# A fused linear-attention, ELU MLP and top-1 expert kernel: expert rows loaded in 32-token blocks and turned on VectorE, and two experts' products interleaved across the seam

## The chip, the cores and the metric

The kernel runs on one core of a Trainium2 chip. The core has five engines with instruction streams of their own that meet only through semaphores: TensorE (PE, matrix products into eight PSUM banks), VectorE (DVE), ScalarE (ACT), GpSimd (POOL) and SyncE (SP, which here issues loads), and 16 DMA engines beside them. The metric is the device time of one launch in microseconds (us), lower is better.

## The reference, cut to what matters

```python
x = attention(r, k, v, w, u)             # linear attention with decay, 2 x 768 tokens, 8 heads x 48
x = elu(x @ w_in) @ w_out                # 1536 tokens, 384 -> 2048 -> 384
logits = x @ w_gate                      # 8 experts
e = argmax(logits); gate = softmax(logits)[e]
# expert e takes its tokens in order, into slots disp[e, 0:384]
h = maximum(einsum('ecd,edf->ecf', disp, w1), 0)     # w1: 8 x 384 x 1024
y = einsum('ecf,efd->ecd', h, w2)                    # w2: 8 x 1024 x 384
out[i] = gate[i] * y[e[i], slot[i]]
```

All is fp32. Products are made from fp32r parts: each operand is split in a rounded part (`_hi`) and the rest (`_lo`), and a product is three matmuls, hi x hi, hi x lo and lo x hi.

## The kernel before

The span has three stages: attention by 128-token chunks; the ELU MLP by six blocks of 256 tokens, in which attention chunks, routing and scatter are woven; and from about 265 us the experts. Routing scatters each token's row (384 values of x, the gate, the token's number) into `slots` in HBM, 384 slots for each expert. An expert computes its first 256 slots; a branch at the end that is not taken with these inputs does the overflow.

Expert 0 runs in an order of its own (tiles of 128 slots, `tile_fc1`, `tile_fc2`, `pick_rows`). Experts 1 to 7 run through `expert(i, r, more)`, one function of that name for each engine; expert 2i+r has its weights in buffer r (`EH[r]`, `EL[r]`; the loaded weights `ER[r]` lie in the same bytes as `EL[r]`), its rows in `xrow[r]`. Experts 2 to 5 are a hardware loop.

TensorE, for f from 0 to 7 (an "f step"): FC1 of 128 hidden features, nine matmuls of 256 columns into `ps_e[f % 2]` (L1718 to L1737), then FC2 of step f-2, six matmuls of 384 columns into the two accumulators `ps_ye` (L1697). FC2 of steps 6 and 7 comes at the end of the expert (L1746), so the next expert begins with three FC1 groups in a row. FC1 of step f waits for ge_lo of step f-2 (L1720). Behind FC2 in step 5 TensorE transposes the next expert's rows, six blocks of 128x128, from `xrow` into `ps_xt` (L1684 to L1695).

ScalarE (L935): ge_hi = relu(ps_e) rounded (L940) in each step; the rounded parts of the next expert's w1 in steps 2 to 4 (L945) and w2 in steps 5 to 7 (L953), 1024 columns each; xe_hi from `ps_xt` in step 5. VectorE (L1296): ge_lo in each step (L1301), the rest of w1 in steps 3 to 5 (L1308), xe_lo (L1293) and the token numbers tok_i (L1315) in step 5; at the end the two products with the gate into `yrow` (L1321). GpSimd: the rest of w2 (L724), then two indirect scatters of `yrow` into `out` (L729).

SP issues the loads from one queue in program order (L546 to L554): for expert e = 2i+r

```python
sp.wait_ge(s_he, ET * (2 * i + r + 1))      # all FC1 of expert e done
load_w(2 * i + 2 + r, r)                    # w1 of expert e+2
sp.wait_ge(s_fc2e, ET * (2 * i + r + 1))    # all FC2 of expert e done
load_w2(2 * i + 2 + r, r)
sp.wait_ge(s_ye[r], 2 * (i + 1))            # yrow of expert e done, xrow free
sp.wait_ge(s_tok[r], i + 1)
load_x(2 * i + 2 + r, r)                    # two DMAs of 128 rows of 386 values
```

Of the kernel before, what the change touches and what calls it, by code (L numbers as in the profile page):

```python
# [12 lines left out]
def build(nc, B, H, S, D, DFF, NE, FE, CAP, rkt_in, nat_in, decay, bonus, bonus_pair, win, wout, wouttr, wgate, wexp, out, slots):  # L13
# [5 lines left out]
    DM = H * D  # L19
# [37 lines left out]
    NOVER = NE + 3  # L57
    LATE = NE * CAP
# [39 lines left out]
    x2t = new("x2t", [128, BT, DM])  # L98
    lg = new("lg", [128, BT, NE])
# [32 lines left out]
    def expert_rows(r):  # L132
        return (new(f"xrow{r}", [128, 2, XR]), new(f"xe_hi{r}", [128, KT, SN], F32R),
                new(f"xe_lo{r}", [128, KT, SN], F32R), new(f"yrow{r}", [128, 2, DM]),
                new(f"tok_i{r}", [128, 2, 1], U32))
# [8 lines left out]
    xrow, xe_hi, xe_lo, yrow, tok_i = zip(rows0, expert_rows(1))  # L144
# [32 lines left out]
    with ctx:  # L177
# [223 lines left out]

        def wait_if(eng, s, count):

            if not (isinstance(count, int) and count <= 0):
                eng.wait_ge(s, count)
# [40 lines left out]
        def _(sp):  # L446
# [128 lines left out]
        def _(pool):  # L575
# [143 lines left out]
            def split_w2(e_i, r):  # L719

                for c in range(N1):
# [25 lines left out]
            split_w2(0, 1)  # L747
# [29 lines left out]
        def _(act):  # L777
# [151 lines left out]
            def expert_x(i, r):  # L929

                act.wait_ge(s_xtr[r], i + 1)
                nc.scalar.copy(xe_hi[r][:, 0:2, :], ps_xt[0][:, :].rearrange("p (k n) -> p k n", k=2)).then_inc(s_xehi[r], 1)
                nc.scalar.copy(xe_hi[r][:, 2, :], ps_xt[1][:, 0:SN]).then_inc(s_xehi[r], 1)
# [48 lines left out]
        def _(dve):  # L982
# [273 lines left out]
            def tokens_of(t, s):  # L1256
                dve.wait_ge(s_xr[0], 16 * (t + 1))
                V.tensor_copy(tok_i[0][:, t, :], xrow[0][:, t, TOKEN:XR]).then_inc(s, 1)

            def gated(t, y):  # L1260
                V.tensor_scalar(yrow[0][:, t, :], y, xrow[0][:, t, GATE:GATE + 1], None, ALU.mult).then_inc(s_ye[0], 1)
# [20 lines left out]
            for c in range(N1):  # L1282
# [4 lines left out]
            dve.wait_ge(s_y0, 1)  # L1287
            gated(0, ps_y[0][:, 0:DM])

            def expert_x(i, r):  # L1290
                for c, (src, dst) in enumerate(((ps_xt[0][:, :], (0, 2)), (ps_xt[1][:, 0:SN], (2, 3)))):
                    dve.wait_ge(s_xehi[r], 2 * i + c + 1)
                    V.tensor_tensor(xe_lo[r][:, dst[0]:dst[1], :], src.rearrange("p (k n) -> p k n", n=SN),  # L1293
                                    xe_hi[r][:, dst[0]:dst[1], :].bitcast(F32), ALU.subtract).then_inc(s_xelo[r], 1)

            def expert(i, r, more):  # L1296
                ni, nr = (i, 1) if r == 0 else (i + 1, 0)
                for f in range(ET):
# [4 lines left out]
                                           op1=ALU.subtract).then_inc(s_gelo, 1)  # L1303
                    if more and F_W1 < f <= F_W1 + N1:
# [11 lines left out]
                for t in range(2):  # L1316
                    if t == 0:
                        dve.wait_ge(s_y0, 2 * i + r + 1)
                    else:
                        dve.wait_ge(s_fc2e, ET * (2 * i + r + 1))  # L1320
                    V.tensor_scalar(yrow[r][:, t, :], ps_ye[t][:, 0:DM], xrow[r][:, t, GATE:GATE + 1], None,  # L1321
                                    ALU.mult).then_inc(s_ye[r], 1)

            tile_row(s_he, ET, s_lrow)
# [39 lines left out]
        def _(pe):  # L1364
# [292 lines left out]
            def pick_rows():  # L1657

                pe.wait_ge(s_xr[0], 32)
                for kt in range(KT):  # L1660
                    mm(ps_s[0][:, 128 * kt:128 * kt + 128], xrow[0][:, 1, 128 * kt:128 * kt + 128], ident[:, :],
# [3 lines left out]
                for kt in range(KT):  # L1665
                    for t in range(BT):
                        last = mm(ps_s[0][:, 128 * kt:128 * kt + 128], rows[:, t, NE + 128 * kt:NE + 128 * kt + 128],
# [16 lines left out]
            def expert_x(i, r):  # L1684
                pe.wait_ge(s_xr[r], 32 * (i + 1))
                if r:
                    pe.wait_ge(s_xelo[0], 2 * (i + 1))
                else:
                    wait_if(pe, s_xelo[1], 2 * i)
                for kt in range(KT):  # L1690
                    for t in range(2):
                        at = (kt % 2) * SN + t * 128
                        last = nc.tensor.transpose(ps_xt[kt // 2][:, at:at + 128],  # L1693
                                                   xrow[r][:, t, 128 * kt:128 * kt + 128], ident[:, :])
                last.then_inc(s_xtr[r], 1)  # L1695

            def fc2_expert(i, r, f, tiles=(0, 1)):  # L1697
                pe.wait_ge(s_gelo, ET * (2 * i + r) + f + 1)
                if f == 0:
                    pe.wait_ge(s_ehi[r], 2 * N1 * (i + 1))  # L1700
                    wait_if(pe, s_elo2[r], N1 * (i + r))
                    y_before, n_before = other(s_ye, r, i)
                    wait_if(pe, y_before, 2 * n_before)
                cols = slice(W1 + f * DM, W1 + (f + 1) * DM)
                for t in tiles:
                    g = slice(t * 128, (t + 1) * 128)
# [7 lines left out]
            def expert(i, r, more):  # L1714
                ni, nr = (i, 1) if r == 0 else (i + 1, 0)

                pe.wait_ge(s_elo1[r], N1 * (i + 1) + (0 if r else N1))
                for f in range(ET):  # L1718
                    q = ET * (2 * i + r) + f
                    wait_if(pe, s_gelo, q if f == 0 else q - 1)  # L1720
# [16 lines left out]
                    last.then_inc(s_he, 1)  # L1737
                    if more and f >= 2:
# [5 lines left out]
                    if more and f == F_X:  # L1744
                        expert_x(ni, nr)
                if more:  # L1746
                    fc2_expert(i, r, ET - 2)
                    fc2_expert(i, r, ET - 1)
                else:
# [12 lines left out]
            expert_x(0, 1)  # L1762
# [114 lines left out]
```

## Time and profile before

| | us |
|---|---|
| median of the timed runs (lowest to highest) | 415.21 (414.87 to 415.24) |
| the profiled execution | 415.56 |
| its span, first to last instruction | 413.7 |
| TensorE busy | 406.2 (98%) |
| VectorE busy | 242.4 (59%) |
| ScalarE busy | 188.1 (45%) |
| GpSimd busy | 231.4 (56%) |
| HBM read and written | 52.0 and 13.2 MB |

The profile is one execution; a row gives when an instruction started, how long it took, its engine, its line in the kernel, and what it wrote from what. "Waited for" is read back from semaphores. Matmuls are pipelined: the next starts while the one before drains, so the distance between starts tells TensorE's rate, and the duration does not.

### The profile page before, as it was taken

How to read it: one execution, taken by the hardware profiler on the slowest of the kernel's cores; microseconds unless marked ns; L12 is line 12 of the kernel's file. 1: busy time of each engine (PE TensorE's matmuls, PEld its weight loads, DVE VectorE, ACT ScalarE, POOL GpSimd, SP SyncE). 2: the span in 40 equal slices, each digit the busy share in tenths (PEclk: the TensorE clock that was granted, in tenths of full speed). 3: DMA queues.
4: the chain of work that ended last, by engine and by line, in shares of the span. 5: the costliest groups of instructions: out<-in, count | busy, mean ns of one | idle time of the engine just before them, and what ended most of it. 6: DMA issues, size and time to landing. Idle time of an engine off the chain costs nothing.

```text
span 413.7 us, 9445 instructions
## 1 busy us (share of the span) xinstructions
PE 406.2 (98%) x3697; PEld 390.3 (94%) x3697; DVE 242.4 (59%) x576; ACT 188.1 (45%) x409; POOL 231.4 (56%) x239
## 2 busy tenths in 40 slices
PE   8999999999999999999999999999999999999995
PEld 8799799999999999999999999999999999999995
DVE  7787955376576547654663487785635546364522
ACT  4786553233333333333343455552645455474420
POOL 3789865567856685668234336065083562826531
PEclk9999999999999999999999999999999999999998
DMA  7998997214030403020018001827383845729000
GB/s 281 399 395 341 348 371 255 72 49 150 10 119 2 139 21 118 2 87 21 2 19 345 2 2 38 326 77 238 135 304 99 346 147 217 279 100 363 8 31 28
DMA packets 18650, 64.98 MB, mean 157 GB/s; under 512 B 2203, under 2 KB 11717, under 8 KB 16432
## 3 DMA queue, kind: packets, MB, share of 16 engines
q1 hardware_dynamic: 16672, 59.67, 39.5%
q0 software_dynamic: 1792, 4.73, 3.0%
q8 instruction: 28, 0.46, 0.5%
q14 instruction: 14, 0.11, 0.1%
q10 hardware_dynamic: 144, 0.00, 0.0%
HBM read 51.98 MB, written 13.21 MB: 158 GB/s over the span
## 4 chain that ended last, share of the span: by engine, by line
PE 88%; DVE 4%; issue 3%; DMA 3%; POOL 1%; ACT 1%; POOLq 0%; SPq 0%; DVEq 0%
PE bank L1369 26%; PE bank L1371 25%; PE bank L1370 24%; PE bank L1390 2%; DMA xrow<-slots 2%; PE bank L1419 1%; PE bank L1455 1%; PE bank L1459 1%; PE bank L1693 1%; PE bank L1448 1%; PE bank L1451 1%; PE bank L1546 1%; PE bank L1728 1%; PE bank L1729 1%; PE bank L1632 1%
## 5 line engine op out<-in xcount | busy, mean ns | idle before, releaser
L707 POOL TENSOR_TENSOR g_lo<-elu,g_hi 128x256 fp32r<-128x256 f32 x95 | 73.7, 777 | 86.9 <-ACT g_hi L882 86.6
L1369 PE MATMUL bank<-xt,wd_hi 128*128 128x256 f32 x285 | 80.5, 283 | 0.6 <-DVE elu L1197 0.6
L1371 PE MATMUL bank<-xt,wd_lo 128*128 128x256 f32 x285 | 80.4, 282 | 0.0
L1370 PE MATMUL bank<-xt,wd_hi 128*128 128x256 f32 x285 | 80.3, 282 | 0.0
L873 ACT ACTIVATE elu<-elu 128x256 f32<-128x256 f32 x96 | 40.1, 418 | 76.4 <-DVE elu L1189 75.9
L1369 PE MATMUL bank<-wd_hi,g_hi 128*128 128x392 f32 (+1 forms) x192 | 67.4, 351 | 0.0
L1371 PE MATMUL bank<-wd_hi,g_lo 128*128 128x392 f32 (+1 forms) x192 | 65.2, 340 | 0.0
L1370 PE MATMUL bank<-wd_lo,g_hi 128*128 128x392 f32 (+1 forms) x192 | 65.1, 339 | 0.0
L1197 DVE SCALAR_TENSOR_TENSOR elu<-elu,bank 128x256 f32<-128x256 f32 x96 | 40.3, 419 | 41.1 <-ACT elu L873 41.1
L882 ACT CAST g_hi<-elu 128x256 fp32r<-128x256 f32 x96 | 39.0, 406 | 44.1 <-DVE elu L1197 44.1
L1369 PEld LDWEIGHTS bank<-xt,wd_hi 128*128 128x128 f32 x285 | 53.9, 189 | 1.2 <-DVE elu L1197 1.1
L1371 PEld LDWEIGHTS bank<-xt,wd_lo 128*128 128x128 f32 x285 | 54.1, 190 | 0.0
L1370 PEld LDWEIGHTS bank<-xt,wd_hi 128*128 128x128 f32 x285 | 54.0, 189 | 0.0
L1301 DVE SCALAR_TENSOR_TENSOR ge_lo<-bank,ge_hi 128x256 fp32r<-128x256 f32 x56 | 23.8, 424 | 48.8 <-ACT ge_hi L940 48.8
L1189 DVE TENSOR_SCALAR elu<-bank 128x256 f32<-128x256 f32 x80 | 33.8, 422 | 31.2 <-PE bank L1371 26.3
L940 ACT ACTIVATE ge_hi<-bank 128x256 fp32r<-128x256 f32 x56 | 21.6, 385 | 53.4 <-PE bank L1371 31.5
L724 POOL TENSOR_TENSOR wd_lo<-wd_raw,wd_hi 128x1024 fp32r<-128x1024 f32 x12 | 30.4, 2559 | 27.5 <-ACT wd_hi L953 24.5
L1369 PEld LDWEIGHTS bank<-wd_hi,g_hi 128*128 128x128 f32 x192 | 36.3, 189 | 2.0 <-POOL g_lo L707 0.8
L724 POOL TENSOR_TENSOR we_lo<-we_raw,we_hi 128x1024 fp32r<-128x1024 f32 x9 | 21.3, 2402 | 27.6 <-ACT we_hi L953 27.6
L1370 PEld LDWEIGHTS bank<-wd_lo,g_hi 128*128 128x128 f32 x192 | 36.4, 190 | 0.0
L1371 PEld LDWEIGHTS bank<-wd_hi,g_lo 128*128 128x128 f32 x192 | 36.0, 188 | 0.0
L729 POOL DMA_INDIRECT out<-yrow,tok_i x16 | 15.7, 982 | 17.4 <-DVE yrow L1321 11.7
(220 smaller groups left out, 943.7 us busy)
## 6 DMA issues: line engine op xcount, KB each, us to landing
we_raw<-wexp SPq DMA_DIRECT2D x8, 1536.0 KB, 6.5
wd_raw<-wexp SPq DMA_DIRECT2D x8, 1536.0 KB, 7.4
rkt<-rkt SPq DMA_DIRECT2D x12, 512.0 KB, 5.7
nat<-nat SPq DMA_DIRECT2D x9, 672.0 KB, 5.4
xrow<-slots SPq DMA_DIRECT2D x16, 193.0 KB, 7.4
wd_raw<-win SPq DMA_DIRECT2D x4, 768.0 KB, 8.6
wd_raw<-wout SPq DMA_DIRECT2D x4, 768.0 KB, 9.0
wo_tr<-wouttr SPq DMA_DIRECT2D x1, 3072.0 KB, 17.6
```

What stands on the lines that cost most here:

```text
L707: nc.gpsimd.tensor_tensor(g_lo[:, f % 4, :], elu[:, f % 2, :], g_hi[:, f % 4, :].bitcast(F32), ALU.subtract).then_inc(s_glo, 1)
L724: nc.gpsimd.tensor_tensor(EL[r][:, cols], ER[r][:, cols], EH[r][:, cols].bitcast(F32), ALU.subtract).then_inc(s_elo2[r], 1)
L729: nc.gpsimd.indirect_dma_start(out=out, out_offset=bass.IndirectOffsetOnAxis(ap=tok_i[r][:, t, :], axis=0), in_=yrow[r][:, t, :], in_offse ...
L873: nc.scalar.activation(elu[:, f % 2, :], elu[:, f % 2, :], ACT.Exp, scale=-1.0 if n == 0 else 1.0).then_inc(s_exp, 1)
L882: nc.scalar.copy(g_hi[:, f % 4, :], elu[:, f % 2, :]).then_inc(s_ghi, 1)
L940: nc.scalar.activation(ge_hi[:, f % 4, :], ps_e[f % 2][:, 0:SN], ACT.Relu).then_inc(s_gehi, 1)
L1189: V.tensor_scalar_min(elu[:, f % 2, :], ps_h[f % 2][:, 0:BN], 0.0).then_inc(s_m, 1)
L1197: V.scalar_tensor_tensor(out=elu[:, f % 2, :], in0=elu[:, f % 2, :], scalar=-1.0, in1=ps_h[f % 2][:, 0:BN], op0=ALU.add, op1=ALU.max).then ...
L1301: V.scalar_tensor_tensor(out=ge_lo[:, f % 4, :], in0=ps_e[f % 2][:, 0:SN], scalar=0.0, in1=ge_hi[:, f % 4, :].bitcast(F32), op0=ALU.max, o ...
L1369: mm(dst, w_hi, x_hi, start=start, stop=False)
L1370: mm(dst, w_hi, x_lo, start=False, stop=False)
L1371: return mm(dst, w_lo, x_hi, start=False, stop=stop)
```

## The change

1. `load_x` no longer loads rows of 386 values with a token on each partition. Four DMAs load, for the partitions 32p to 32p+31, columns 96p to 96p+95 of the 256 rows in eight blocks of 32 rows (1024 pieces of 384 bytes in all); a fifth loads gate and token number (256 pieces of 8 bytes).
2. VectorE turns these blocks of 32x32 with one `transpose` of 128x768 into `xcol` (the bytes of `x2t`), in step 4; ScalarE and VectorE split xe_hi and xe_lo from there in step 5. The six TensorE transposes of each expert go. A partition then holds feature 3p+kt, not 128kt+p, so w1's rows are permuted on the host (`thirds`), and expert 0's transposes and `pick_rows` read every third column (`block_cols`).
3. In SP's queue `load_x` moves ahead of `load_w`, waiting only for `s_tok`; the wait for `yrow` goes, since the gate is now copied out of `xrow` beside tok_i (a maximum of the column with itself).
4. FC2 of an expert's steps 6 and 7 moves behind FC1 of steps 0 and 1 of the next expert; the products with the gate (`expert_out`) move behind ge_lo of step 1 of the next.
5. FC2 waits for w2 by chunks of 1024 columns, and for the old expert's two accumulators one by one.
6. Of expert 1's splits, the third chunk of w1 moves from VectorE to GpSimd and the third chunk of w2 from GpSimd to VectorE, in step 1.

```diff
+        def block_cols(rows, kt):
+            return rows.rearrange("p (m k) -> p k m", k=KT)[:, kt, :]
+        def xrow_blocks(r):
+            return xrow[r][:, :, :].rearrange("p t c -> p (t c)")[:, 0:2 * DM].rearrange("p (b c) -> p b c", b=8)
             def load_x(e, r):
-                for t in range(2):
-                    sp.dma_start(xrow[r][:, t, :],
-                                 slots[bass.ds(e * CAP + t * 128, 128), :]).then_inc(s_xr[r], 16)
+                for p in range(4):
+                    sp.dma_start(xrow_blocks(r)[32 * p:32 * p + 32, :, :],
+                                 slots[bass.ds(e * CAP, SN), 96 * p:96 * p + 96]
+                                 .rearrange("(b i) c -> i b c", i=32)).then_inc(s_xr[r], 16)
+                sp.dma_start(xrow_gt(r), slots[bass.ds(e * CAP, SN), GATE:XR]
+                             .rearrange("(t p) c -> p t c", t=2)).then_inc(s_xr[r], 16)
...
                 for r in range(2):
+                    sp.wait_ge(s_tok[r], i + 1)
+                    load_x(2 * i + 2 + r, r)
                     sp.wait_ge(s_he, ET * (2 * i + r + 1))
                     load_w(2 * i + 2 + r, r)
                     sp.wait_ge(s_fc2e, ET * (2 * i + r + 1))
                     load_w2(2 * i + 2 + r, r)
-                    sp.wait_ge(s_ye[r], 2 * (i + 1))
-                    sp.wait_ge(s_tok[r], i + 1)
-                    load_x(2 * i + 2 + r, r)
...
-            split_w2(0, 1)
+            split_w1_last()
+            split_w2(0, 1, N1 - 1)
...
-            for c in range(N1):
+            for c in range(N1 - 1):
                 dve.wait_ge(s_ehi[1], c + 1)
...
+            def expert_cols(i, r):
+                dve.wait_ge(s_xr[r], rows_loaded(i, r))
+                V.transpose(xcol.rearrange("p k (b n) -> p b k n", n=32),
+                            xrow_blocks(r).rearrange("p b (n k) -> p b k n", k=KT)).then_inc(s_xtr[r], 1)
+            def expert_out(i, r):
+                dve.wait_ge(s_tok[r], i + 1)
+                for t in range(2):
+                    if t == 0:
+                        dve.wait_ge(s_y0, 2 * i + r + 1)
+                    else:
+                        dve.wait_ge(s_fc2e, ET * (2 * i + r + 1))
+                    V.tensor_scalar(yrow[r][:, t, :], ps_ye[t][:, 0:DM], gate[r][:, t, :], None, ALU.mult).then_inc(s_ye[r], 1)
...
+                    if f == 1 and behind:
+                        expert_out(bi, br)
+                    if f == 1 and not behind:
+                        dve.wait_ge(s_ehi[1], 2 * N1)
+                        dve.wait_ge(s_elo2[1], N1 - 1)
+                        cols = slice(W1 + (N1 - 1) * ECH, W1 + N1 * ECH)
+                        V.tensor_tensor(EL[1][:, cols], ER[1][:, cols], EH[1][:, cols].bitcast(F32),
+                                        ALU.subtract).then_inc(s_elo2[1], 1)
...
+                    if more and f == F_X - 1:
+                        expert_cols(ni, nr)
                     if more and f == F_X:
                         expert_x(ni, nr)
                     if f == 5:
-                        dve.wait_ge(s_xr[r], 32 * (i + 1))
+                        dve.wait_ge(s_xr[r], rows_loaded(i, r))
                         wait_if(dve, s_sout[r], 32 * i)
-                        V.tensor_copy(tok_i[r][:, :, :], xrow[r][:, :, TOKEN:XR]).then_inc(s_tok[r], 1)
+                        V.tensor_tensor(gate[r][:, :, :], xrow_gt(r)[:, :, 0:1], xrow_gt(r)[:, :, 0:1], ALU.max)
+                        V.tensor_copy(tok_i[r][:, :, :], xrow_gt(r)[:, :, 1:2]).then_inc(s_tok[r], 1)
...
+            expert_cols(0, 1)
             tile_row(s_he, ET, s_lrow)
...
-            def expert_x(i, r):
-                pe.wait_ge(s_xr[r], 32 * (i + 1))
...
+                if w2_chunk(f) > w2_chunk(f - 1):
+                    pe.wait_ge(s_ehi[r], 2 * N1 * (i + 1) - N1 + w2_chunk(f))
+                    wait_if(pe, s_elo2[r], N1 * (i + r) - N1 + w2_chunk(f))
...
+                    if f < 2 and behind:
+                        fc2_expert(bi, br, ET - 2 + f)
                     if more and f >= 2:
                         fc2_expert(i, r, f - 2)
...
-                    if more and f == F_X:
-                        expert_x(ni, nr)
-                if more:
-                    fc2_expert(i, r, ET - 2)
-                    fc2_expert(i, r, ET - 1)
```

## Rows read from the trace of the kernel before

**Rows 1.** The page: span, busy time of each engine, granted clock by slice.

```profile
span 413.7 us, 9445 instructions
PE 406.2 (98%) x3697; PEld 390.3 (94%) x3697; DVE 242.4 (59%) x576; ACT 188.1 (45%) x409; POOL 231.4 (56%) x239
...
PEclk9999999999999999999999999999999999999998
```

**Rows 2.** Timeline, TensorE: start us, us, engine, line, operation; experts 1, 2, 7.

```profile
285.85 0.28 PE L1728 MATMUL bank<-xe_hi,wd_hi 128*128 128x256 f32 x1
...
286.90 0.28 PE L1369 MATMUL bank<-xe_hi,wd_hi 128*128 128x256 f32 x1
...
305.59 0.38 PE L1369 MATMUL bank<-xe_hi,we_hi 128*128 128x256 f32 x1
...
391.91 0.28 PE L1728 MATMUL bank<-xe_hi,wd_hi 128*128 128x256 f32 x1
```

**Rows 3.** Timeline, VectorE, steps 3 and 4 of expert 2.

```profile
309.48 0.42 DVE L1301 SCALAR_TENSOR_TENSOR ge_lo<-bank,ge_hi 128x256 fp32r<-128x256 f32 x1 [1.69 <-ACT ge_hi L940]
309.82 1.22 DVE L1308 TENSOR_TENSOR wd_lo<-wd_raw,wd_hi 128x1024 fp32r<-128x1024 f32 x1
311.58 0.42 DVE L1301 SCALAR_TENSOR_TENSOR ge_lo<-bank,ge_hi 128x256 fp32r<-128x256 f32 x1 [0.54 <-ACT ge_hi L940]
```

**Rows 4.** Timeline, TensorE, the transposes of one expert's rows (six groups like it).

```profile
314.11 0.81 PE L1693 MATMUL bank<-ident,xrow 128*128 128x128 f32 x6
```

**Rows 5.** Waits from 286 us on: us in total, times, longest us.

```profile
PEld bank L1693 <- DMA xrow<-slots: 0.6, 2, 0.4
```

**Rows 6.** Timeline, VectorE, before expert 1.

```profile
280.15 0.69 DVE L1249 TENSOR_SCALAR hrow<-bank 128x512 f32<-128x512 f32 x1 [1.23 <-PE bank L1371]
```

**Rows 7.** Groups of VectorE by form, 300 to 414 us: count, busy us, mean ns.

```profile
L1293 DVE TENSOR_TENSOR xe_lo<-bank,xe_hi 128x512 fp32r<-128x512 f32 x5 | 3.5, 691 | 2.2 <-ACT xe_hi L932 2.2
```

**Rows 8.** Timeline, VectorE, tok_i of expert 0's second half.

```profile
283.87 0.14 DVE L1258 CAST tok_i<-xrow 128x1 uint32<-128x1 f32 x1
```

**Rows 9.** Timeline, TensorE, the picks of expert 0.

```profile
268.97 1.50 PE L1667 MATMUL bank<-picked,x2row 128*128 128x128 f32 x12
```

**Rows 10.** DMA issues by window (272 to 372 us): count, KB each, us to landing.

```profile
xrow<-slots SPq DMA_DIRECT2D x2, 193.0 KB, 2.6
...
we_raw<-wexp SPq DMA_DIRECT2D x1, 1536.0 KB, 6.1
...
wd_raw<-wexp SPq DMA_DIRECT2D x1, 1536.0 KB, 6.6
...
we_raw<-wexp SPq DMA_DIRECT2D x1, 1536.0 KB, 6.2
...
wd_raw<-wexp SPq DMA_DIRECT2D x1, 1536.0 KB, 6.5
...
wd_raw<-wexp SPq DMA_DIRECT2D x1, 1536.0 KB, 7.7
```

**Rows 11.** Timeline, SP: the issue of single DMAs and of two x loads.

```profile
2.21 0.43 SPq L462 DMA_DIRECT2D nat<-nat  x1
2.69 0.43 SPq L465 DMA_DIRECT2D nat<-nat  x1
...
280.33 0.35 SPq L516 DMA_DIRECT2D we_raw<-wexp  x1
...
374.97 0.86 SPq L523 DMA_DIRECT2D xrow<-slots  x2
```

**Rows 12.** Timeline, ScalarE: steps 0 and 5 of expert 1, step 2 of 3.

```profile
287.10 0.38 ACT L940 ACTIVATE ge_hi<-bank 128x256 fp32r<-128x256 f32 x1 [4.10 <-PE bank L1732]
...
295.65 0.38 ACT L940 ACTIVATE ge_hi<-bank 128x256 fp32r<-128x256 f32 x1 [0.77 <-PE bank L1371]
...
324.83 1.04 ACT L945 CAST we_hi<-we_raw 128x1024 fp32r<-128x1024 f32 x1
```

**Rows 13.** Stretches: us, busy by engine, PEclk, DMA share, GB/s; x rows alone.

```profile
274.00:276.50 2.50, 2.50 (x15) 2.27 (x14) 2.50 (x2) 0.77 (x1) 2.50 (x1) 1.00 0.54 156
```

More of the change, by code:

```diff
@@ L134, in expert_rows @@
                 new(f"xe_lo{r}", [128, KT, SN], F32R), new(f"yrow{r}", [128, 2, DM]),
-                new(f"tok_i{r}", [128, 2, 1], U32))
+                new(f"tok_i{r}", [128, 2, 1], U32), new(f"gate{r}", [128, 2, 1]))
     wo_at = top[0]
@@ L143, in build @@
     ge_lo = new("ge_lo", [128, 4, SN], F32R)
-    xrow, xe_hi, xe_lo, yrow, tok_i = zip(rows0, expert_rows(1))
+    xrow, xe_hi, xe_lo, yrow, tok_i, gate = zip(rows0, expert_rows(1))
     wo_tr, end_g = put("wo_tr", [128, KT, DFF], F32, wo_at)
@@ L717, in _, with split_w1_last, split_w2 @@
                 scatter_rows(NB - 1, t)
-            def split_w2(e_i, r):
-                for c in range(N1):
+            def split_w1_last():
+                pool.wait_ge(s_ehi[1], N1)
+                cols = slice((N1 - 1) * ECH, N1 * ECH)
+                nc.gpsimd.tensor_tensor(EL[1][:, cols], ER[1][:, cols], EH[1][:, cols].bitcast(F32),
+                                        ALU.subtract).then_inc(s_elo1[1], 1)
+            def split_w2(e_i, r, chunks=N1):
+                for c in range(chunks):
                     pool.wait_ge(s_ehi[r], 2 * N1 * e_i + N1 + c + 1)
@@ L1312, in expert @@
                     if f == 5:
-                        dve.wait_ge(s_xr[r], 32 * (i + 1))
+                        dve.wait_ge(s_xr[r], rows_loaded(i, r))
                         wait_if(dve, s_sout[r], 32 * i)
-                        V.tensor_copy(tok_i[r][:, :, :], xrow[r][:, :, TOKEN:XR]).then_inc(s_tok[r], 1)
[L1316 to L1322, printed above, removed]
+                        V.tensor_tensor(gate[r][:, :, :], xrow_gt(r)[:, :, 0:1], xrow_gt(r)[:, :, 0:1], ALU.max)
+                        V.tensor_copy(tok_i[r][:, :, :], xrow_gt(r)[:, :, 1:2]).then_inc(s_tok[r], 1)
+                if not more:
+                    expert_out(i, r)
+            expert_cols(0, 1)
             tile_row(s_he, ET, s_lrow)
@@ L1666, in pick_rows @@
                     for t in range(BT):
[L1667 removed]
+                        last = mm(ps_s[0][:, 128 * kt:128 * kt + 128], block_cols(rows[:, t, NE:NE + DM], kt),
                                   picked[:, t, :], start=False, stop=kt == KT - 1 and t == BT - 1,
@@ L1682, in _, with w2_chunk @@
             last.then_inc(s_y0, 1)
-            def expert_x(i, r):
-                pe.wait_ge(s_xr[r], 32 * (i + 1))
[L1686 to L1695, printed above, removed]
+            def w2_chunk(f):
+                return -(-(f + 1) * DM // ECH)
             def fc2_expert(i, r, f, tiles=(0, 1)):
                 pe.wait_ge(s_gelo, ET * (2 * i + r) + f + 1)
[L1699 to L1703, printed above, removed]
+                if w2_chunk(f) > w2_chunk(f - 1):
+                    pe.wait_ge(s_ehi[r], 2 * N1 * (i + 1) - N1 + w2_chunk(f))
+                    wait_if(pe, s_elo2[r], N1 * (i + r) - N1 + w2_chunk(f))
                 cols = slice(W1 + f * DM, W1 + (f + 1) * DM)
                 for t in tiles:
+                    if f == 0:
+                        y_before, n_before = other(s_ye, r, i)
+                        pe.wait_ge(y_before, 2 * n_before - 1 + t)
                     g = slice(t * 128, (t + 1) * 128)
@@ L1712, in fc2_expert, with expert @@
                     last.then_inc(s_fc2e, 1)
-            def expert(i, r, more):
+            def expert(i, r, more, behind):
                 ni, nr = (i, 1) if r == 0 else (i + 1, 0)
+                bi, br = (i - 1, 1) if r == 0 else (i, 0)
                 pe.wait_ge(s_elo1[r], N1 * (i + 1) + (0 if r else N1))
@@ L1743, in expert @@
                                 fc2_expert(i, r, f - 2 - t, (t,))
-                    if more and f == F_X:
-                        expert_x(ni, nr)
-                if more:
-                    fc2_expert(i, r, ET - 2)
-                    fc2_expert(i, r, ET - 1)
-                else:
+                if not more:
                     for t in range(2):
@@ L1850 @@
     w_in = moe_w_in[order].reshape(DM // 128, 128, DFF // 128, 128).transpose(1, 2, 0, 3).reshape(128, -1)
+    thirds = [DM // 128 * p + kt for kt in range(DM // 128) for p in range(128)]
     gate_pad = np.zeros((DM, 32), np.float32)
@@ L1867 @@
         "wexp": np.ascontiguousarray(np.stack(
-            [np.concatenate([tiled(moe2_w1[e]), tiled(moe2_w2[e])], axis=1) for e in list(range(NE)) + [0]])),
+            [np.concatenate([tiled(moe2_w1[e][thirds]), tiled(moe2_w2[e])], axis=1) for e in list(range(NE)) + [0]])),
     }
```

54 lines of the change are left out of this document (31 added, 23 removed).

## The prediction, made before the changed kernel ran

> **What bounds the kernel now.** I read the page first: 413.7 us of span in a profiled execution of 415.56 us, TensorE busy 98% at full granted clock [rows 1]. The median of the timed runs is 415.21, 0.35 below that execution; I make the sum as a difference inside the span and put it on 415.2. The change touches expert 1 onward, so I read the PE timeline there. The first FC1 matmul of expert 1 starts at 285.85 and that of expert 7 at 391.91 [rows 2]: 106.06 us for six experts, 17.68 each. VectorE's ge_lo follows TensorE from one f step to the next at 309.48 and 311.58 [rows 3], so a step of nine FC1 and six FC2 matmuls takes 2.10, and eight take 16.80. The other 0.88 per expert is what TensorE does besides: six transposes of the next expert's rows (0.81 by the row, the drain of the last one included) [rows 4], a gap at the second FC1 group of each expert, where TensorE catches up with the ge_lo chain because the seam has no FC2 to put between (the stretched 0.38 us matmul) [rows 2], and, twice, 0.6 us in all, the landing of those rows [rows 5]. There is no other idle time: this stage is bound by TensorE's own work, and only work taken off it counts, as long as nothing else becomes slower than 16.80 per expert.
>
> **Removed.** The transposes (L1693), their wait for xrow and the seam gap all go for the six periods from expert 1 to expert 7: 106.06 - 6 x 16.80 = 5.26 us. At the seam FC1 of the new expert now alternates with the last two FC2 of the old, so ge_lo of one step has three groups, 3.1 us, to come in, against one group (285.85 to 286.90, 1.05) [rows 2] before, and I take the gap as gone. The seventh group of transposes, before expert 1, I count at nothing: behind it TensorE transposes hrow, which VectorE has ready at 280.84 (280.15 + 0.69) [rows 6], just where that work starts.
>
> **Added on VectorE.** The block transpose is not in the trace of before. Nearest rows: 0.69 us for 512 elements and 1.22 for 1024, so 0.96 for 768 at one element a cycle [rows 3, 7]. Upper bound: twice the time, 1.9, if it drains or reads (a stride of three elements) at half rate. I take 0.96, since all fp32 rows of VectorE that I looked at lie on that line. The gate copy costs 0.15, like the tok_i copy [rows 8]. The two gate products move from the end of the expert to behind step 1 of the next. The first needs the old expert's first accumulator, done 0.5 before that FC2 group ends, the second the end of it; behind them there wait on VectorE only ge_lo of step 2, and on TensorE the first FC2 of the new expert, a whole FC1 group (1.05) later: at two times 0.6 us (384 elements by the same line) hidden, and what they cost without that cover is 0.6 per expert. VectorE is busy 59% of the span [rows 1], so as a sum all this fits; as a chain it must be looked at, below.
>
> **The other edits.** FC2 now waits for w2 chunk by chunk: it only loosens. Expert 1's third w1 chunk goes to GpSimd and its third w2 chunk to VectorE at step 1, where 1.22 us delays ge_lo of step 2 by about 0.3 us against a cover of 2: nothing. The early transposes and pick_rows read rows with a stride of three elements on TensorE; the largest group, on the path, takes 1.50 us at present [rows 9]: between nothing and a doubling (1.5). I take nothing, since what they compute and stream is the same, and keep some of the rest in the range. VectorE turns expert 1's rows ahead of hrow: the two present loads are issued at 273 and land after 2.6 us [rows 10]; five take 1.5 us more to issue, so they land near 277.5 and the transpose is over by 278.5, before hrow at 280.15 [rows 6].
>
> **What takes the place of the wait: the load queue.** This is where the argument turns. load_x moves in SP's queue from behind w2 to ahead of w1, and grows from two DMAs to five. It waits for tok_i, the last thing VectorE does in step 5. So SP's w1 load of expert e+2 is now queued behind tok_i of expert e and five issues. Two issues take 0.86; and in a run of single ones the next starts 0.48 later [rows 11]: five take about 2.3. w1 lands 6.1, 6.6, 6.2, 6.5, 6.2 and 7.7 after its issue in the six loads of the stage (one row stands for both of 6.2) [rows 10], a median of 6.35. ScalarE reads it in step 2 of the next expert, VectorE after that, and tok_i of that expert comes behind both. That closes a ring, which I follow once, each instruction starting about 0.08 before the end of the one ahead on its engine:
> - landing to ge_lo of step 3: w1 chunk on ScalarE 1.04, ge_hi 0.38, ge_lo 0.42 [rows 3, 12], less overlap of 0.05: 1.79;
> - on VectorE then three w1 chunks (3.66), two ge_lo (0.84), the transpose 0.96, xe_lo 1.1 (0.69 and 0.42), gate and tok_i 0.3 [rows 3, 7, 8], less nine overlaps (0.72): 6.14;
> - the signal to SP 0.2, taken like that from TensorE to ScalarE (286.90 to 287.10) [rows 2, 12], five issues 2.3, w1 lands 6.35.
> The sum is 16.78 us a round, against 16.80 of TensorE's. So at my values the ring just keeps pace, with no room: each further us in any member of it costs one us in each of five rounds.
> It also starts late. tok_i of expert 0 ends at 284.01 [rows 8], so w1 of expert 2, now issued at 280.33 [rows 11], is issued at 286.5 and lands at 292.84. TensorE's FC1 of step 5 of expert 1, whose ge_hi starts at 295.65, must begin at 294.40 (295.65 - 0.2 - 1.05) [rows 12] and wants ge_lo of step 3; the first FC1 of expert 2, at 285.85 + 14.7 = 300.6 in the new order, wants ge_lo of step 6. Going back 1.79 from the one, and 1.79 + 6.14 + 0.34 (ge_lo of step 6) from the other, w1 should land by 292.6 and 292.3. So it is 0.6 late, once. w2's load goes out two groups (2.1 us) later, 4.4 us into the next expert; were it as slow as w1's slowest (7.7) it would be there at 12.1, and ScalarE reads it behind ge_hi and xe_hi of step 5, at about 13: nothing, or as much as it lands beyond 13.
>
> **Sum.** -5.26 + 0.6 + 5 x 0 = -4.7 with landings of 6.35. With their mean of 6.55, 0.2 more at the start and 0.18 in each of five rounds: -3.6. I take a value nearer to the first, -4.3: 410.9 us.
>
> **Small packets, weighed.** The x rows of one expert, 256 packets of 1.5 KB alone in the queue, take 0.54 of 2.5 us, 1.35 us of all engines [rows 13]. They become 1024 packets of 384 bytes and 256 of 8 bytes. If time goes by bytes nothing is left of them when w1 starts, 2.3 us later; if it goes by packets they take 5.4 or more and hold w1 up by 5.4 - 2.3 = 3.1. I take the first: the loads are spread over the five issues.
> The Trainium skill, in DMA: Bandwidth & Descriptors, Specifications, wants transfers of at least 512 bytes for full rate and says that smaller ones cost a read-modify-write. By it, as an estimate of doubled packet time, the rows would take 2.7 us and hold w1 up by 0.4, and the sum would be some 2 us worse, -2.5; no row here shows a packet of this size by itself.
> On the stride, the skill's page SBUF — State Buffer, under Door 1: The DMA port swizzle, says that full bandwidth needs at least two hits in each 16-byte line, yet also that a stride of four fp32 is free. The first half would bring the half-rate case of the next part; no row of before shows it.
>
> **Rivals.**
> 1. *No ring* (VectorE or the landings a little quicker than I reckon, as in the 6.1 and 6.2 rows): the whole 5.26 and up to 0.5 of the start: 409.4 to 410.2. Chance 0.15.
> 2. *The ring bites partly* (small packets by the skill's rule, issues of 0.48, landings as at 7.7): a round of 17.0 to 17.4, hence 412.0 to 414.3. Chance 0.21.
> 3. *Slower than before: the turning at half rate.* A transpose of 1.9 makes the round 17.7: five rounds of 0.9, 1.6 at the start, 6.1 against 5.26: 416.0. It decides from about 0.8 added to the round (six times 0.8 is 4.8, with the first 0.6 equal to the gain). For it speaks the unseen instruction and its stride, against it that fp32 rows of VectorE lie on one line. Between 1.2 and 1.9 it falls in rival 2 or at no change. Chance 0.13.
> 4. *Packets by count*: 3.1 on every round, -5.26 + 3.7 + 5 x 3.07 = +13.8: 429. Against it: the first load of these rows lands in 2.6 us, most of it fixed. Chance 0.04.
> 5. *It doesn't do what it says*: the strided reads on TensorE cost their upper 1.5, or the seam keeps its gap (0.15 in each of six): 412 to 413. Chance 0.05.
>
> **From these to the numbers.** The forecast, a ring that about keeps pace (410.2 to 412.0), has 0.42. Range: rivals 1, 2 and 5 and the near part of 3: 409.4 to 415.2, which leaves out rather under 2 in 10. About 0.2% (0.83 us) is what a measurement of this kernel can tell from no change: faster means under 414.4. Faster 0.42 + 0.15 + 0.20 + 0.04 = 0.81; within 0.2% 0.08 (parts of 2, 3 and 5); slower 0.11.
>
> **What the profile after would show.** No transposes on PE between 286 and 400, and the first FC1 matmuls of experts 1 and 7 some 101 to 102 us apart. A VectorE transpose of 128x768 at 0.9 to 1.0. SP's w1 issues some 1.5 us after FC1 of step 7 instead of 0.3, behind five x loads of 0.43. ScalarE's first w1 copy (we_hi or wd_hi) waiting 1 to 1.5 us for DMA in each expert, and PE gaps in step 5 and at the seam only where that wait grows from expert to expert. Wrong it would be if the transpose took over 1.3, or w1 landed over 7 us after its issue; then the gaps stand in every expert and of one size.

## The result, and the profile of the changed kernel

| | before | after |
|---|---|---|
| median of the timed runs, us (lowest to highest) | 415.14 (414.87 to 415.24) | 430.67 (430.46 to 431.08) |
| span of the profiled execution, us | 413.7 | 428.9 |
| TensorE busy | 406.2 (98%) | 407.9 (95%) |

The ratio is 1.0376, with a 95% interval of 1.0365 to 1.0387: slower by 3.8%, where I had forecast 1% faster, and far outside my range. The head of the page (busy us and share of each engine, the granted clock in 40 slices) and two pieces of its chain that ended last answer to [rows 1]:

```profile
span 428.9 us, 9451 instructions
PE 407.9 (95%) x3655; PEld 390.2 (91%) x3655; DVE 260.9 (61%) x592; ACT 187.2 (44%) x409; POOL 232.7 (54%) x239
...
PEclk9999999999999999999999999999899999899999
...
PE bank L1417 18%; PE bank L1419 17%; PE bank L1418 17%; DMA we_raw<-wexp 5%; DMA wd_raw<-wexp 3%; PE bank L1438 2%; DVE we_lo L1356 2%; SPq L537 2%; DVE gate L1365 1%; DVE xe_lo L1323 1%; PE bank L1467 1%; DVE x2t L1317 1%; POOL g_lo L723 1%; PE bank L1503 1%; DVE ge_lo L1341 1%
```

The chain no longer stays on TensorE. It runs through the w1 loads (8% of the span), the issue of the x rows on SP (L537), VectorE's splits, the transpose (x2t L1317) and the gate copy (L1365): the members of the ring that the prediction followed once around. VectorE's busy time rose by 18.5 us. The TensorE timeline (start us, duration us) at the first FC1 matmul of experts 1, 2 and 7, and at step 5 of expert 1, answers to [rows 2]:

```profile
287.05 0.28 PE L1768 MATMUL bank<-xe_hi,wd_hi 128*128 128x256 f32 x1
...
298.18 0.38 PE L1417 MATMUL bank<-xe_hi,wd_hi 128*128 128x256 f32 x1 [2.41 <-DVE ge_lo L1341]
...
307.01 0.38 PE L1768 MATMUL bank<-xe_hi,we_hi 128*128 128x256 f32 x1 [2.24 <-DVE ge_lo L1341]
...
404.98 0.36 PE L1768 MATMUL bank<-xe_hi,wd_hi 128*128 128x256 f32 x1 [2.23 <-issue]
```

Where the 15.2 us of span came from: expert 1 begins 1.20 later (287.05 against 285.85 in [rows 2]); experts 1 to 6 take 117.93 us in place of 106.06, +11.87; what follows takes 23.92 against 21.79, +2.13, which is the two FC2 groups of 1.05 that moved there. In the new order TensorE needs 14.7 us for expert 1 (two FC2 groups fewer) and 16.80 for each of the next five, 98.7. So 19.2 us of the 117.93 are not matmuls at their usual pace. Some 16 of them TensorE stands still: 2.58 ahead of step 5 of expert 1, 1.1 to 2.4 just ahead of each new expert (11.8 for the six), and about 1.5 in small waits. The other 3.3 are two stretches in which its clock was down (stretch, us, busy us and count of PE, PEld, DVE, ACT and POOL, granted clock, DMA share, GB/s):

```profile
307.60:311.00 3.40, 3.40 (x16) 3.40 (x15) 0.42 (x1) 0.38 (x1) 3.40 (x2) 0.51 0.89 163
365.60:369.20 3.60, 3.52 (x14) 3.52 (x15) 0.78 (x3) 0.38 (x1) 3.60 (x2) 0.53 0.62 120
```

A granted clock of 0.51 is the 1.2 GHz level, of 2.4 GHz in full. TensorE had stood 2.40 and 2.33 us just before, yet gaps as long ahead of 346.12 and 404.98 were not followed by such a stretch. It cost no time here: the rounds of the ring below that hold a slow stretch take 19.60 and 19.58, the three others 19.51 to 19.68.

The timeline of VectorE in the second half of expert 1 answers to [rows 3] and shows the surprise:

```profile
298.04 1.22 DVE L1356 TENSOR_TENSOR we_lo<-we_raw,we_hi 128x1024 fp32r<-128x1024 f32 x1
...
300.64 1.21 DVE L1317 STREAM_TRANSPOSE x2t<-xrow 128x768 f32<-128x768 f32 x1
...
303.21 1.01 DVE L1323 TENSOR_TENSOR xe_lo<-x2t,xe_hi 128x512 fp32r<-128x512 f32 x2
304.15 2.32 DVE L1365 TENSOR_TENSOR gate<-xrow 128x2 f32<-128x2 f32 x1
306.39 0.15 DVE L1366 CAST tok_i<-xrow 128x2 uint32<-128x2 f32 x1
```

The gate copy, two elements for each partition, takes 2.32 us. The tile view of `gate` (minimum, median and maximum ns) shows that it is so in nearly every expert, but not in expert 0:

```profile
L1365 DVE TENSOR_TENSOR gate<-xrow x7: 150/2323/2365, 304.2 to 417.1; 128x2 f32<-128x2 f32 x7
L1281 DVE TENSOR_TENSOR gate<-xrow x2: 148/150/151, 273.8 to 285.1; 128x1 f32<-128x1 f32 x2
```

The one at 417.05 that took 0.15 is expert 7's, with no later expert's w2 to be split. GpSimd's timeline has, beside the slow one of expert 1:

```profile
303.85 4.93 POOL L746 TENSOR_TENSOR we_lo<-we_raw,we_hi 128x1024 fp32r<-128x1024 f32 x2 [14.72 <-ACT we_hi L976]
```

Two chunks of GpSimd's split of the next w2, about 2.5 us each, the first from 303.85 to about 306.3; the copy, started 0.30 after it, ends at 306.47.

**The ring, member by member.** From tok_i of expert 1 (306.39) to that of expert 2 (325.99) it is 19.60 us, and the next four are 19.5 to 19.7. SP's and ScalarE's timelines between:

```profile
306.74 1.84 SPq L537 DMA_DIRECT2D xrow<-slots  x4
308.76 0.40 SPq L540 DMA_DIRECT2D xrow<-slots  x1
309.43 0.35 SPq L530 DMA_DIRECT2D wd_raw<-wexp  x1
...
315.78 1.05 ACT L968 CAST wd_hi<-wd_raw 128x1024 fp32r<-128x1024 f32 x1 [1.29 <-DMA wd_raw<-wexp]
```

| member of the ring | prediction | measured |
|---|---|---|
| tok_i's end to the first x issue | 0.2 | 0.20 (306.54 to 306.74) |
| five x issues, to the w1 issue | 2.3 | 2.69 (to 309.43) |
| w1 issue to ScalarE's first copy | 6.35 | 6.35 (to 315.78) |
| splits, transpose, xe_lo, gate, tok_i | 1.79 + 6.14 | 10.36 (to 326.14) |
| round | 16.78 | 19.60 |

Of the 2.43 in the last member the gate copy is 2.20 (2.35 at 323.72 against 0.15) and the transpose 0.25.

### The profile page after: what moved, and what is told of

It reads as the page before. It is cut to its first block, busy times and chain, and to the rows that moved or that the text cites. A ratio compares the mean times of both kernels' runs of the same rounds, so it can differ in the third digit from the quotient of the medians.

```text
span 428.9 us, 9451 instructions
## 1 busy us (share of the span) xinstructions
PE 407.9 (95%) x3655; PEld 390.2 (91%) x3655; DVE 260.9 (61%) x592; ACT 187.2 (44%) x409; POOL 232.7 (54%) x239
## 4 chain that ended last, share of the span: by engine, by line
PE 62%; DVE 12%; DMA 8%; issue 8%; POOL 4%; SPq 3%; ACT 2%; DVEq 0%; POOLq 0%; ACTq 0%
PE bank L1417 18%; PE bank L1419 17%; PE bank L1418 17%; DMA we_raw<-wexp 5%; DMA wd_raw<-wexp 3%; PE bank L1438 2%; DVE we_lo L1356 2%; SPq L537 2%; DVE gate L1365 1%; DVE xe_lo L1323 1%; PE bank L1467 1%; DVE x2t L1317 1%; POOL g_lo L723 1%; PE bank L1503 1%; DVE ge_lo L1341 1%
## 5 line engine op out<-in xcount | busy, mean ns | idle before, releaser
L1341 DVE SCALAR_TENSOR_TENSOR ge_lo<-bank,ge_hi 128x256 fp32r<-128x256 f32 x56 | 22.8, 415 | 57.8 <-ACT ge_hi L963 57.7
L746 POOL TENSOR_TENSOR wd_lo<-wd_raw,wd_hi 128x1024 fp32r<-128x1024 f32 x11 | 27.6, 2532 | 24.0 <-ACT wd_hi L976 24.0
```

The costliest lines, as they stand in the source:

```text
L746: nc.gpsimd.tensor_tensor(EL[r][:, cols], ER[r][:, cols], EH[r][:, cols].bitcast(F32), ALU.subtract).then_inc(s_elo2[r], 1)
L1341: V.scalar_tensor_tensor(out=ge_lo[:, f % 4, :], in0=ps_e[f % 2][:, 0:SN], scalar=0.0, in1=ge_hi[:, f % 4, :].bitcast(F32), op0=ALU.max, o ...
```

## The experiments

My theory after this result: VectorE's copy waits until a running GpSimd instruction ends, and the ring passes those 2.2 us on to every round. Rivals: the two-source form of the copy, or its place on VectorE, is slow by itself; or the queue order alone makes the loss.

**The copy with one source.**

```diff
-V.tensor_tensor(gate[r][:, :, :], xrow_gt(r)[:, :, 0:1], xrow_gt(r)[:, :, 0:1], ALU.max)
+V.tensor_copy(gate[r][:, :, :], xrow_gt(r)[:, :, 0:1])
```

> The changed kernel with the gate copied by a one-source copy in place of the maximum of the column with itself. Theory A (ring: the two-source gate copy of step 5 waits about 2.2 us for GpSimd's w2 split, and stands in the ring tok_i -> x loads -> w1 load -> splits -> tok_i): the copy takes 0.15, a round falls from 19.6 to 17.4, and 5 rounds x 2.17 plus about 2.4 of expert 1 come back: 417.4 us. Theory B (the small packets ahead of w1, or the five issues, make the time; the gate copy only fills VectorE's idle time): not under 428.

Measured: 431.62 us (ratio 1.0403, interval 1.0368 to 1.0437), not 417.4. The rows of VectorE and GpSimd:

```profile
303.42 2.33 DVE L1365 COPY gate<-xrow 128x2 f32<-128x2 f32 x1
```

```profile
303.13 4.92 POOL L746 TENSOR_TENSOR we_lo<-we_raw,we_hi 128x1024 fp32r<-128x1024 f32 x2 [14.47 <-ACT we_hi L976]
```

The copy still takes 2.33, so my 0.15 for it was wrong: the wait does not hang on two sources, and the instruction can be a plain copy.

**w1 ahead of the x rows in SP's queue**, the rest as changed, and then the same with the one-source copy.

```diff
-sp.wait_ge(s_tok[r], i + 1)
-load_x(2 * i + 2 + r, r)
 sp.wait_ge(s_he, ET * (2 * i + r + 1))
 load_w(2 * i + 2 + r, r)
+sp.wait_ge(s_tok[r], i + 1)
+load_x(2 * i + 2 + r, r)
```

> The changed kernel with SP's order changed: the w1 load ahead of the wait for tok_i and of the five x loads. The two-source gate copy stays. Theory A: the ring is cut, but the gate copy still ends with GpSimd's first w2 chunk and holds ge_lo of step 6, by 0.8 to 0.9 us in each of six experts: 416 us. Theory B (small packets or issues ahead of w1 are all there is): the whole gain is seen, 411 us. If the order doesn't matter: 430.

> Both edits: one-source gate copy and w1 ahead of the x loads. Theory A: no ring and no held ge_lo, 16.8 us per expert: before minus 5.3 for the transposes and the seam, plus 1.2 for the strided reads of expert 0's rows: 411.1 us. If VectorE's work as such (transpose 1.21, gate products behind step 1) were too much, 413 or more with gaps on TensorE in steps 5 to 7.

Measured: 417.47 us (412.92 to 418.29; ratio 1.0046, interval 1.0022 to 1.0069) and 415.37 (412.82 to 418.99; 1.0004, 0.997 to 1.0038). Opening the ring takes away 13 us at once. The copy now starts 0.27 to 0.29 us behind the recorded start of GpSimd's split, which is just where it turns whether it is held. In the profiled executions, both at the fast end of their runs (412.9 and 412.8), one of the six copies that meet a split was held: expert 1's in e2, expert 3's in e3 (maximum 2357 ns, median 173), with a PE gap of 1.14 behind it. That the number of held copies differs from one execution to the next, and makes the wide spread, is my reading; the other executions were not profiled. I had expected 416 and 411.1; of the 4.9 between them 2.1 were measured, less than either spread. With the copy held in one expert in both forms, the form of the copy settles nothing.

**The gate copy alone moved to step 3**, tok_i left in step 5.

> The changed kernel with the two-source gate copy kept, but moved from behind xe_lo in step 5 to step 3, where GpSimd isn't splitting. Theory A (it waits for GpSimd): 0.15 us each, and the time of the one-source copy, 417.4 us. Rival (the two-source form of this column of 8-byte pieces takes 2.3 us wherever it stands): 2.3 us each at step 3 and about 430 us.

Measured: 429.66 (1.0334, 1.0298 to 1.0369), not 417.4. The gate copies take 0.151 each, and:

```profile
303.88 2.34 DVE L1367 CAST tok_i<-xrow 128x2 uint32<-128x2 f32 x1
```

The 2.3 us have passed to the next instruction, whose duration in the kernel before was 0.16. So it is the moment that is slow, not the gate's operands.

**Gate and tok_i moved ahead of xe_lo**, in step 5.

> The changed kernel with gate and tok_i copied in step 5, but ahead of xe_lo: the ring stays closed, only the wait for GpSimd and the 0.94 us of xe_lo leave it. Theory A: a round is 19.6 - 2.2 - 0.9 = 16.5, under TensorE's 16.8, so only expert 1's late w1 is left (2.6 to 2.9 us): 414 us. If moving it only hands the wait to xe_lo, which reads SBUF too and now meets GpSimd: about 430 as before. If the ring were no ring: 411.

Measured: 422.65 (418.79 to 423.77; 1.018, 1.0163 to 1.0198), between the 414 and the 430 of my two cases. VectorE and GpSimd in expert 2 of the profiled execution, which was the fastest, at 418.79:

```profile
320.91 0.16 DVE L1364 CAST tok_i<-xrow 128x2 uint32<-128x2 f32 x1
320.98 3.23 DVE L1323 TENSOR_TENSOR xe_lo<-x2t,xe_hi 128x512 fp32r<-128x512 f32 x2
324.13 0.74 DVE L1341 SCALAR_TENSOR_TENSOR ge_lo<-bank,ge_hi 128x256 fp32r<-128x256 f32 x2
```

```profile
321.49 4.97 POOL L746 TENSOR_TENSOR wd_lo<-wd_raw,wd_hi 128x1024 fp32r<-128x1024 f32 x2 [6.90 <-ACT wd_hi L976]
```

The pair of xe_lo takes 3.23 in place of 1.03. The wait is out of the ring, but ge_lo of step 6 stands behind xe_lo, and the PE gaps at the first three seams stay (2.43, 1.07 and 1.14). In the last three experts xe_lo took 1.02 to 1.04 and no gap stood; I take it that the slower executions had more experts like the first three, but none was profiled. It is the third kind of VectorE instruction that GpSimd's split holds. ge_lo, which reads PSUM, runs beside the same split in 0.37 each.

**GpSimd held back instead**: VectorE's program is untouched; GpSimd gets one wait ahead of each split, here those of the loop.

```diff
...
+pool.wait_ge(s_tok[0], i + 1)
 split_w2(i, 1)
 scatter_out(i, 0)
+pool.wait_ge(s_tok[1], i + 1)
 split_w2(i + 1, 0)
...
```

> The changed kernel (430.67 us) with one wait added and nothing else: GpSimd starts its split of the next expert's w2 (L746) only when tok_i of the running expert is written, some 0.3 us later than now. VectorE's program, its operands and SP's order stay. If the gate copy takes 2.3 us because GpSimd's split runs beside it, both copies take 0.15 in every expert, the round falls from 19.6 to about 17.4, and the time is 418 to 420 (five rounds of 2.2, 11 us, off; the transpose of 1.21, the issues of 2.7 and the late w1 of expert 2 stay). If the copy is slow for a reason of its own (its operands' places, what VectorE did before it), it takes 2.3 again and the time is 430 to 431.

Measured: 417.23 us (416.85 to 418.9; 1.0057, 1.0043 to 1.0071), 0.8 under the 418 to 420 that I expected, since I had counted the 2.2 in five rounds and not the sixth. The tile view of `gate`, and tok_i of two experts:

```profile
L1369 DVE TENSOR_TENSOR gate<-xrow x7: 152/156/167, 303.8 to 403.5; 128x2 f32<-128x2 f32 x7
...
303.90 0.17 DVE L1370 CAST tok_i<-xrow 128x2 uint32<-128x2 f32 x1
...
390.80 0.17 DVE L1370 CAST tok_i<-xrow 128x2 uint32<-128x2 f32 x1
```

and GpSimd's split behind it, with expert 1:

```profile
304.16 7.12 POOL L746 TENSOR_TENSOR we_lo<-we_raw,we_hi 128x1024 fp32r<-128x1024 f32 x3 [15.22 <-DVE tok_i L1370]
```

All seven copies take 0.15 to 0.17, and a start of GpSimd 0.3 us later gives back 13.4 us: six waits of 2.2. This settles the cause. It also weighs the rest of the ring: 86.90 us for five rounds, 17.38 each, which is my 16.78 with the transpose (0.25) and the issues (0.39) at their measured size, 17.42.

**Both copies in step 3**, ahead of the w1 chunk, SP's order as changed; then the same with w1 first in SP's queue.

```diff
+if f == 3:
+    dve.wait_ge(s_xr[r], rows_loaded(i, r))
+    wait_if(dve, s_sout[r], 32 * i)
+    V.tensor_tensor(gate[r][:, :, :], xrow_gt(r)[:, :, 0:1], xrow_gt(r)[:, :, 0:1], ALU.max)
+    V.tensor_copy(tok_i[r][:, :, :], xrow_gt(r)[:, :, 1:2]).then_inc(s_tok[r], 1)
... (the same four lines go from step 5)
```

> The changed kernel with gate and tok_i copied in step 3 instead of behind xe_lo in step 5, SP's order as changed (x loads, then w1). Theory A (ring through tok_i, lengthened by a wait for GpSimd): both are gone. Copies of 0.15, w1 issued 0.3 us after the last FC1 again, 16.8 us per expert: 415.3 - 5.3 + 1.2 = 411.2 us, all runs within 1 us. If the x packets ahead of w1 or the order of the queue cost something by themselves: 413 or more.

> The changed kernel with gate and tok_i copied in step 3 ahead of the w1 chunk (as in e5_tok_early, 414.84 us), and in SP's queue w1 of expert e+2 ahead of that expert's x rows. If what was left in e5 is the late w1 of expert 2 (issued at 288.34 behind tok_i of expert 0 and five x loads; PE gap of 2.59 in step 5 of expert 1), the gap goes, w1 of expert 2 is issued near 281.5 and the time is 412.2. If that gap has another cause (the splits of expert 1 on VectorE or GpSimd), it stays and the time is 414.8.

Measured: e5 414.84 us (0.9986, 0.9976 to 0.9995), 3.6 over what I expected. The copies take 0.15, experts 2 to 6 take 16.80 each, but expert 1 does not:

```profile
287.67 0.40 SPq L540 DMA_DIRECT2D xrow<-slots  x1
288.34 0.36 SPq L530 DMA_DIRECT2D we_raw<-wexp  x1
288.89 0.35 SPq L533 DMA_DIRECT2D we_raw<-wexp  x1
```

w1 of expert 2 is still queued behind tok_i of expert 0 and five x issues, and w2 follows 0.55 behind it into the same DMA engines. TensorE stands 2.58 before 298.32, and expert 1 takes 19.10 (287.18 to 306.28) in place of 14.7. The gap is not all of it; behind it comes a stretch like the two in the changed kernel (columns as there):

```profile
299.40:302.70 3.30, 3.30 (x15) 3.30 (x14) 3.30 (x6) 1.38 (x3) 0.00 (x0) 0.50 0.58 120
```

3.3 us at half the granted clock cost 1.6, and with the ring open nothing hides them. This profiled execution was the slowest of ten (415.9; the mean granted clock was 0.993 in it and in two more of 415.6 and 415.7; the five at 1.0 took 414.3 to 414.9). With w1 first it is issued at 281.34, expert 1 takes 14.85 (286.89 to 301.74) with no gap and no slow stretch, and the time is 411.24 (0.9908, 0.9892 to 0.9925), 1 below what I expected, since I had taken one gap for the whole. In e6, below, whose profiled execution kept its full clock, expert 1 takes 17.90, 3.05 over e9: 2.67 in the gap, the rest at the next seam and in the restarts. Another 0.4 is between the two series of runs, by the kernel before in each (415.51 and 415.14).

**Expert 0 without strided reads**: w1 of expert 0 also in its old row order, as a tenth entry of `wexp`; the transposes and `pick_rows` read 128 adjacent columns. First on e5, then on e9.

```diff
...
-block_cols(xrow[0][:, 1, 0:DM], kt)
+xrow[0][:, 1, 128 * kt:128 * kt + 128]
...
```

> The same, and expert 0 gets its own, unpermuted w1 and its rows are read by TensorE in runs instead of every third column. If the strided reads are what expert 1 starts 1.2 us later for: 410.0 us. If the start is late for another reason (five x issues, the transpose ahead of hrow): 411.2.

> As e9, and expert 0 with w1 rows of its own in the old order, so that TensorE reads expert 0's rows without the stride of three (as in e6_tok_plain0, 413.13 us). If the gap of 2.6 and the strided reads (1.7) are all that was left, the time is 410.5, and TensorE does from expert 1 to expert 7 six times 16.80 us. If the two overlap, 411 to 412.

Measured: 413.13 us (0.9945, 0.9928 to 0.9961), 3.1 over the 410.0 that I expected, since e5's gap stays in it (2.67 ahead of 296.74); and 410.29 (410.1 to 410.47; 0.9886, 0.9869 to 0.9902), where I expected 410.5. The groups of weight loads (count, busy us, mean ns), of the changed kernel and then of e10:

```profile
L1715 PEld LDWEIGHTS bank<-picked,x2row 128*128 128x128 f32 x12 | 2.2, 262 | 0.0
L1709 PEld LDWEIGHTS bank<-ident,xrow 128*128 128x128 f32 x6 | 1.2, 260 | 0.0
```

```profile
L1715 PEld LDWEIGHTS bank<-picked,x2row 128*128 128x128 f32 x12 | 1.4, 192 | 0.0
L1709 PEld LDWEIGHTS bank<-ident,xrow 128*128 128x128 f32 x6 | 0.8, 191 | 0.1
```

The stride of 12 bytes adds a third to each weight load, and expert 1 starts 1.04 later for it (286.89 in e9, 285.85 in e10). In e10 TensorE takes 98.86 us from expert 1 to expert 7, against 98.7 reckoned:

```profile
285.85 0.28 PE L1768 MATMUL bank<-xe_hi,wd_hi 128*128 128x256 f32 x1
...
384.71 0.28 PE L1768 MATMUL bank<-xe_hi,wd_hi 128*128 128x256 f32 x1
```

**The transpose over runs.** As e10, with each block of 96 columns read in three runs of 32 adjacent values and w1's rows permuted to match. The overflow branch, not taken here, keeps the old order and would be wrong.

```diff
-xrow_blocks(r).rearrange("p b (n k) -> p b k n", k=KT)
+xrow_blocks(r).rearrange("p b (k n) -> p b k n", k=KT)
```

> As e10, with the block transpose reading runs of 32 contiguous values in place of every third value (w1's rows permuted to match; the branch for the overflow, not taken here, keeps the other order, so that branch would be wrong). If the transpose's 1.21 us against 0.96 comes of the stride, it takes 0.96 here; if it is the transpose's own rate, 1.21 again. VectorE has room in every expert, so the time is that of e10 by both, 410.5.

Measured: 410.17 us (409.55 to 410.22; 0.9878, 0.9861 to 0.9894), as e10. The transposes of e10, then of e11:

```profile
L1317 DVE STREAM_TRANSPOSE x2t<-xrow 128x768 f32<-128x768 f32 x6 | 7.3, 1208 | 0.0
```

```profile
L1317 DVE STREAM_TRANSPOSE x2t<-xrow 128x768 f32<-128x768 f32 x6 | 5.8, 970 | 0.0
```

The transpose itself runs at the 0.96 that I gave it; the stride of three elements adds 0.24. VectorE has room for either when the ring is open.

**The kernel before, with its tok_i copy one step later** (step 6).

> The kernel before with one line moved: its one-source tok_i copy goes from step 5 to step 6, behind ge_lo, where GpSimd is in its w2 split. If any VectorE instruction that works from SBUF alone may wait for GpSimd's running one: copies of 1 to 2.4 us in place of 0.16 in part or all of the seven; time between unchanged and +1.2 us for each that waits. If it was something of the changed kernel's layout: 0.16 everywhere and the time unchanged.

Measured: 415.5 (0.9998, 0.9988 to 1.0008), and

```profile
L1315 DVE CAST tok_i<-xrow x7: 158/1854/1862, 300.0 to 403.8; 128x2 uint32<-128x2 f32 x7
```

So the wait is no property of the changed kernel: in the kernel before, too, the copy takes 1.85 when GpSimd is in its split. There it holds nobody up. The kernel before kept clear of it by 0.34 us, with the start of tok_i at 298.91 and that of GpSimd's split at 299.25.

## Why the prediction was wrong, step by step

- **Removed: right.** The transposes and the seam gap were worth 5.26, and e10, where nothing takes their place, has 408.5 of span against 413.7: -5.2. Against the kernel before as it ran beside e10 (415.14) the median is 4.85 lower.
- **The ring: the right mechanism, two members mis-sized.** The chain, its landing time (6.35 in the round shown, 6.35 to 6.6 in all five) and its signal were right to 0.2 us. The five issues took 2.69, not 2.3: +0.39. The transpose took 1.21 against 0.96: +0.25, by the stride. Alone these two would have given rounds of 17.4, the top of rival 2: e12 has 17.38.
- **The gate copy: the step that failed.** I priced it at 0.15 from tok_i of expert 0 [rows 8], where GpSimd runs no split, and put it into step 5, where GpSimd does, without looking at what GpSimd had under way at that moment: a wait of one engine for the other has no place anywhere in its sum. It cost 2.2 in six experts, 13.2 us, two thirds of the miss of 19.8. My two signs of being wrong, a transpose over 1.3 or w1 landing over 7 us after its issue in every expert, did not come (1.21, and 6.35 to 6.6 but for one load); the gaps at the seams did, and of another cause. I had said of the ring that each further us counts five times, and priced its smallest member from one row taken elsewhere. The Trainium skill has the rule, in SBUF — State Buffer, Who interferes with whom: VectorE and GpSimd share a pair of SBUF ports under an exclusive lock, taken by VectorE instructions with two SBUF inputs against a GpSimd one that reads SBUF, and by copies and casts in their two-port mode; who comes second waits for the whole instruction. All four slow kinds here agree (gate copy in either form, tok_i, xe_lo; in which mode the copies ran no row shows), and so does ge_lo, with its one SBUF input, in not being held.
- **The late start of expert 1: mis-sized.** I gave it 0.6. w1 of expert 2 was issued at 288.19 and not 286.5, since tok_i of expert 0 came 1.2 later (the strided reads) and the issues took longer; and it took 8.1 to land, with w2, free at once, issued 0.55 behind it; in e9, where w2 follows 6.6 us behind, the same load took 6.3. I had put w2 4.4 us into the expert, which holds only from expert 2 on. In the changed kernel TensorE stands 2.58 before 298.18 for it. From e5 to e9 the medians fall by 3.6, of which 3.05 is this load by expert 1 of e6 and e9.
- **Strided reads: wrong.** I took nothing, between 0 and 1.5; expert 1 began 1.2 later (1.04 from e9 to e10; the group of [rows 9] takes 2.26 against 1.50, the one before it 1.15 against 0.83), with a third more in each of their weight loads.
- **Small packets (rival 4): its 429 was near the time, its mechanism false.** The DMA view from 272 to 412 us (count, KB, median us to landing) has the x rows at

```profile
xrow<-slots SPq DMA_DIRECT2D x28, 96.0 KB, 2.3
...
xrow<-slots SPq DMA_DIRECT2D x7, 2.0 KB, 2.2
```

  ahead of w1 loads of 6.3 to 6.6, no slower than those of [rows 10]. So it was luck that this number came near. The estimate of +0.4 that I took from the Trainium skill's rule on transfers under 512 bytes is not seen.
- **Right at nothing:** the seventh group of transposes (TensorE waits 0.78 us for hrow where it stood), and the gate products behind ge_lo of step 1, beside which e10's TensorE keeps its 16.80.
- **Rival 3** asked the right question, what if something adds over 0.8 to a round, and looked for it only in the transpose.

The terms again, at their measured size: -5.26, strided reads +1.2, late start of expert 1 +2.6, six copies held +13.2, five rounds at 17.4 +3.0: +14.7, against +15.2 in the span.

## What to carry to other kernels

Price a small instruction by what runs on the neighbouring engine at the moment where it will stand, not by the same instruction elsewhere: here one of 0.15 us took 2.3 beside GpSimd's split, and cost 13 us in the end. Before a load is queued behind a consumer's signal, follow the ring it closes, and keep the long load (w1) ahead of the one that waits (x rows). A gain that does not show is worth isolating: with the two copies in step 3, w1 first and expert 0 read without a stride, the same change is 1.1% faster than the kernel before (410.29), and at 410.17 with the turned runs.

## What the runs showed of the hardware that I had not expected

- A VectorE copy, cast or two-input instruction on SBUF that starts while GpSimd runs a `tensor_tensor` of 128x1024 is held until that one ends (2.3 us for a copy of 0.15). The hand-over is decided within hundredths of a us: in e3 a copy 0.27 us behind the recorded start of GpSimd's instruction ran in 0.18 (317.08 against 316.81) and one 0.29 behind in 0.16 (300.30 against 300.01), while another 0.29 behind was held (333.90 against 333.61). In e7 the second half of xe_lo was held where it started 0.09 behind (321.58 against 321.49), so no one distance is the rule.
- GpSimd waits too. Its first instruction of a split takes 2.40 us where it starts behind both copies (e12), 2.60 to 2.64 in the changed kernel, where it starts while VectorE's xe_lo still runs and the copy comes after it, and 2.80 to 2.81 in e3 where the copies got in first. I read it as GpSimd, already started by its record, waiting for xe_lo to end, and the copy and GpSimd then contending for what it lets go; no run separates that.
- TensorE's granted clock fell to the 1.2 GHz level for some 3.4 us behind some gaps of 2.3 to 2.6 us and not behind others of that length. It was hidden in the ring of the changed kernel and cost 1.6 in e5.
- An fp32 stride of 12 bytes is not free: 1.21 against 0.97 us in the VectorE transpose, 262 against 192 ns in TensorE's weight load. The Trainium skill's page SBUF — State Buffer, under Door 1: The DMA port swizzle, calls strides up to four fp32 free; for this stride of three the measurement decides against it.
